# A mixture of experts on one core: the first quarter of the next slot's weights is split in two pieces between the copies of h

## The reference

```python
# x: 2304 x 512, w1: 8 x 512 x 1024, w2: 8 x 1024 x 512
logits = x @ w_gate
e_idx = np.argmax(logits, axis=1)          # one expert for each token
gate_w, eom = ...                          # a factor for each token
for e in range(8):
    mask = e_idx == e
    h = np.maximum(x[mask] @ w1[e], 0.0)
    out[mask] = gate_w[mask, None] * eom[mask, e, None] * (h @ w2[e])
```

## Time and profile before

| | |
|---|---|
| median of 3 runs | 1075.23 us (1075.14 to 1076.69) |
| the profiled execution | 1075.23 us, its span 1073.4 us |
| TensorE's mean granted clock in it | 0.982 of full speed |
| busy: PE, DVE, ACT, POOL | 95%, 57%, 56%, 43% of the span |
| third stage: slot 0 starts, slot 1 starts, last slot starts | 780.87, 796.05, 1052.14 us |

### The profile page before, as it was taken

The page is one execution under the profiler, slowest core; times in us unless marked ns, Lnnn a source line. Parts: engine busy times, 40 slices in busy tenths (PEclk is TensorE's granted clock), DMA queues, the critical chain, the costliest instruction groups (busy, mean ns, idle before and its releaser), DMA issues. The chain is left out here.

```text
span 1073.4 us, 19432 instructions
## 1 busy us (share of the span) xinstructions
PE 1017.6 (95%) x6901; PEld 840.3 (78%) x6901; DVE 612.5 (57%) x1137; ACT 596.3 (56%) x902; POOL 461.1 (43%) x725
## 2 busy tenths in 40 slices
PE   7999999999998999999999999999299999999996
PEld 5778778778776888888888888899177777777774
DVE  5788788888784334222422422332757777777773
ACT  4777787777774334222322322233168888877773
POOL 4777777777772000000000000000347777777773
PEclk9999999999999999999999999999589999999999
DMA  4322322323112110000000000010981554510110
GB/s 111 83 51 69 82 51 77 74 63 77 39 28 71 49 40 1 20 20 1 10 20 10 0 20 20 1 31 11 349 326 39 198 209 172 193 39 32 40 39 33
DMA packets 78891, 75.16 MB, mean 70 GB/s; under 512 B 49103, under 2 KB 59855, under 8 KB 78802
## 3 DMA queue, kind: packets, MB, share of 16 engines
q1 hardware_dynamic: 75282, 63.49, 19.7%
q0 software_dynamic: 3520, 10.49, 3.0%
HBM read 64.52 MB, written 10.49 MB: 70 GB/s over the span
## 5 line engine op out<-in xcount | busy, mean ns | idle before, releaser
L915 DVE TENSOR_TENSOR g_buf<-r_buf 128x512 f32<-128x512 f32 (+1 forms) x80 | 51.1, 639 | 236.1 <-ACT r_buf L853 236.1
L1165 POOL MEMSET ones<- 128x128 bf16 x1 | 0.2, 210 | 416.0 <-POOLq L652 416.0
L853 ACT ACTIVATE r_buf<-h_ps 128x512 f32<-128x512 f32 (+1 forms) x80 | 44.4, 556 | 240.0 <-PE h_ps L799 240.0
L1328 ACT ACTIVATE w_hi<-w_experts 128x2048 fp32r x88 | 161.1, 1906 | 13.2 <-issue 13.2
L1102 POOL TENSOR_TENSOR w_lo<-w_experts,w_hi 128x2048 fp32r<-128x2048 f32 x22 | 138.8, 6307 | 64.5 <-ACT w_hi L1328 64.5
L1102 DVE TENSOR_TENSOR w_lo<-w_experts,w_hi 128x2048 fp32r<-128x2048 f32 x66 | 149.1, 2286 | 28.0 <-ACT w_hi L1328 28.0
L478 ACT ACTIVATE e_sb<-s_sb,stats,live 128x576 f32<-128x576 f32 x144 | 124.5, 865 | 22.4 <-POOL stats L264 21.0
L799 PE MATMUL h_ps<-x_hi,w_in_hi 128*128 128x512 f32 (+1 forms) x320 | 120.2, 376 | 2.3 <-DVE x_lo L901 2.3
L799 PE MATMUL h_ps<-x_hi,w_in_lo 128*128 128x512 f32 (+1 forms) x320 | 118.6, 371 | 0.0
L799 PE MATMUL h_ps<-x_lo,w_in_hi 128*128 128x512 f32 (+1 forms) x320 | 118.5, 370 | 0.0
L816 PE MATMUL y_ps<-g_hi,w_out_hi 128*128 128x512 f32 (+1 forms) x320 | 117.9, 368 | 0.0
(11 more groups left out here) (190 smaller groups left out, 2228.3 us busy)
## 6 DMA issues: line engine op xcount, KB each, us to landing
w_experts<-in_moe_w_dram SPq DMA_DIRECT2D x16, 2048.0 KB, 9.6
y_rows<-y_row SPq DMA_DIRECT2D x36, 128.0 KB, 2.4
k_raw<-in_k_dram SPq DMA_DIRECT2D x32, 128.0 KB, 3.1
q_raw<-in_q_dram SPq DMA_DIRECT2D x32, 128.0 KB, 2.9
w_raw<-in_moe_w_in_dram SPq DMA_DIRECT2D x16, 256.0 KB, 3.1
v_nat<-in_v_dram SPq DMA_DIRECT2D x16, 256.0 KB, 2.6
y_T<-in_moe_w_out_dram SPq DMA_DIRECT2D x16, 256.0 KB, 2.6
v_odd<-in_v_dram SPq DMA_DIRECT2D x16, 64.0 KB, 2.3
```

What stands on the lines that cost most here:

```text
L915: V.tensor_tensor(g_buf[:, 0:cols], r_buf[:, 0:cols], r_buf[:, 0:cols], ALU.mult).then_inc(sq_done, 1)
L1328: nc.scalar.activation(group_of(w_hi, g), raw_group(buf, g), ACT.Copy).then_inc(hi_done, 1)
```

## The change

Group 0 is cut into two pieces of 128 x 1024 (blocks 0 and 1, blocks 2 and 3), so a slot's weights have five parts instead of four. On ScalarE the high part of piece 0 is made between the first relu and the copy of the first half of h, that of piece 1 between this copy and the second relu; groups 1 and 2 stay behind the copies, group 3 in front of the next slot's relu. On VectorE the low part of piece 0 is made right behind the low part of the first half of h, that of piece 1 where group 0 was. The waits count parts; TensorE's first products wait for both pieces. Its transposes of the second half of h go in front of the 5th product of group 2 instead of the 4th; those of the first half keep their place.

```diff
+PARTS = ((0, 0, 2), (0, 2, 4), (1, 0, 4), (2, 0, 4), (3, 0, 4))
+NPARTS = len(PARTS)
...
-        def split_lo(eng, alu, t, g, buf, done):
-            eng.wait_ge(hi_done, 4 * t + g + 1)
-            alu.tensor_tensor(group_of(w_lo, g), raw_group(buf, g), group_of(w_hi, g).bitcast(F32),
-                              ALU.subtract).then_inc(done, 1)
+        def split_lo(eng, alu, t, part, buf, done):
+            g, c0, c1 = PARTS[part]
+            eng.wait_ge(hi_done, NPARTS * t + part + 1)
+            alu.tensor_tensor(group_of(w_lo, g)[:, c0:c1], raw_group(buf, g)[:, c0:c1],
+                              group_of(w_hi, g)[:, c0:c1].bitcast(F32), ALU.subtract).then_inc(done, 1)
...
                 for g in range(2):
-                    pe.wait_ge(lo_dve, 3 * t + g + 2)
+                    pe.wait_ge(lo_dve, (NPARTS - 1) * t + g + 3)
-                    products(h_ps[g][:], x_hi, x_lo, 0, g, ahead_of=2 if g else None,
+                    products(h_ps[g][:], x_hi, x_lo, 0, g, ahead_of=6 if g else None,
                              between=lambda: h_transposed(t, 0)).then_inc(he_done, 1)
...
-                    products(oe_ps[p][:], h_hi, h_lo, 4 * g, 2 + g, ahead_of=None if g else 1,
+                    products(oe_ps[p][:], h_hi, h_lo, 4 * g, 2 + g, ahead_of=None if g else 4,
                              between=lambda: h_transposed(t, 1)).then_inc(y_done, 1)
...
-            def split_w(t, g, weights):
+            def split_w(t, part, weights):
                 buf, need = weights
-                if g % 2 == 0:
+                g, c0, c1 = PARTS[part]
+                if c0 == 0 and g % 2 == 0:
                     wait_first(act, w1_ready if g == 0 else w2_ready, need, act_on)
                 if not static(t) or t >= 1:
                     act.wait_ge(he_done if g < 2 else y_done, 2 * t - 1 + g % 2)
-                nc.scalar.activation(group_of(w_hi, g), raw_group(buf, g), ACT.Copy).then_inc(hi_done, 1)
+                nc.scalar.activation(group_of(w_hi, g)[:, c0:c1], raw_group(buf, g)[:, c0:c1], ACT.Copy).then_inc(hi_done, 1)
...
                 relu(t, 0)
+                if more:
+                    split_w(t + 1, 0, following)
                 split_h(t, 0)
+                if more:
+                    split_w(t + 1, 1, following)
                 relu(t, 1)
                 if more:
                     split_x(t + 1)
                 split_h(t, 1)
                 if more:
-                    split_w(t + 1, 0, following)
-                    split_w(t + 1, 1, following)
                     split_w(t + 1, 2, following)
+                    split_w(t + 1, 3, following)
...
                 split_h(t, 0)
                 if more:
+                    buf = weight_buffer(dve, t + 1)
+                    split_lo(dve, nc.vector, t + 1, 0, buf, lo_dve)
                     split_x(t + 1)
                 split_h(t, 1)
                 if more:
-                    buf = weight_buffer(dve, t + 1)
-                    split_lo(dve, nc.vector, t + 1, 0, buf, lo_dve)
                     split_lo(dve, nc.vector, t + 1, 1, buf, lo_dve)
+                    split_lo(dve, nc.vector, t + 1, 2, buf, lo_dve)
                 scale(t, p)
                 if more:
-                    split_lo(dve, nc.vector, t + 1, 2, buf, lo_dve)
+                    split_lo(dve, nc.vector, t + 1, 3, buf, lo_dve)
```

More of the change, by code:

```diff
@@ L1115, in load @@
                     end = sp.value_load(control[0:1, ENDS + e - BUFS:ENDS + e - BUFS + 1], min_val=0, max_val=SLOTS)
-                    wait_first(sp, lo_dve, 3 * end + 1, sp_on)
+                    wait_first(sp, lo_dve, (NPARTS - 1) * end + 1, sp_on)
                     wait_first(sp, lo_pool, end + 1, sp_on)
@@ L1162, in split @@
                 buf = weight_buffer(pool, t)
-                split_lo(pool, nc.gpsimd, t, 3, buf, lo_pool)
+                split_lo(pool, nc.gpsimd, t, NPARTS - 1, buf, lo_pool)
             nc.gpsimd.memset(ones[:], 1.0).then_inc(pool_set, 1)
@@ L1236, in products @@
                 for c in range(4):
-                    if c == ahead_of:
-                        between()
                     w = [x[:, g, c * 512:(c + 1) * 512] for x in (w_hi, w_lo)]
                     for n, (lhs, rhs) in enumerate(((lhs_hi, w[0]), (lhs_hi, w[1]), (lhs_lo, w[0]))):
+                        if 3 * c + n == ahead_of:
+                            between()
                         last = pe.matmul(out, lhs[:, c0 + c, :], rhs, start=(g != 3 and c == 0 and n == 0),
@@ L1268, in output @@
                     if g == 0:
-                        pe.wait_ge(lo_dve, 3 * t + 4)
+                        pe.wait_ge(lo_dve, (NPARTS - 1) * (t + 1) + 1)
                     else:
                         pe.wait_ge(lo_pool, t + 2)
-                    products(oe_ps[p][:], h_hi, h_lo, 4 * g, 2 + g, ahead_of=None if g else 1,
+                    products(oe_ps[p][:], h_hi, h_lo, 4 * g, 2 + g, ahead_of=None if g else 4,
                              between=lambda: h_transposed(t, 1)).then_inc(y_done, 1)
@@ L1327, in split_w @@
                     act.wait_ge(he_done if g < 2 else y_done, 2 * t - 1 + g % 2)
-                nc.scalar.activation(group_of(w_hi, g), raw_group(buf, g), ACT.Copy).then_inc(hi_done, 1)
+                nc.scalar.activation(group_of(w_hi, g)[:, c0:c1], raw_group(buf, g)[:, c0:c1], ACT.Copy).then_inc(hi_done, 1)
             def slot(t, first, more):
                 if not first:
-                    split_w(t, 3, (weight_buffer(act, t), None))
+                    split_w(t, 4, (weight_buffer(act, t), None))
                 if more:
@@ L1341, in slot @@
                 if more:
-                    split_w(t + 1, 0, following)
-                    split_w(t + 1, 1, following)
                     split_w(t + 1, 2, following)
+                    split_w(t + 1, 3, following)
             act.wait_ge(control_done, 1)
             weights = weights_of(0)
-            split_w(0, 0, weights)
-            split_w(0, 1, weights)
+            for part in range(3):
+                split_w(0, part, weights)
             split_x(0)
-            split_w(0, 2, weights)
-            split_w(0, 3, weights)
+            for part in range(3, NPARTS):
+                split_w(0, part, weights)
             slot(0, True, True)
@@ L1466, in slot @@
                 if more:
-                    buf = weight_buffer(dve, t + 1)
-                    split_lo(dve, nc.vector, t + 1, 0, buf, lo_dve)
                     split_lo(dve, nc.vector, t + 1, 1, buf, lo_dve)
+                    split_lo(dve, nc.vector, t + 1, 2, buf, lo_dve)
                 scale(t, p)
                 if more:
-                    split_lo(dve, nc.vector, t + 1, 2, buf, lo_dve)
+                    split_lo(dve, nc.vector, t + 1, 3, buf, lo_dve)
             buf = weight_buffer(dve, 0)
-            split_lo(dve, nc.vector, 0, 0, buf, lo_dve)
-            split_lo(dve, nc.vector, 0, 1, buf, lo_dve)
+            for part in range(3):
+                split_lo(dve, nc.vector, 0, part, buf, lo_dve)
             split_x(0)
-            split_lo(dve, nc.vector, 0, 2, buf, lo_dve)
+            split_lo(dve, nc.vector, 0, 3, buf, lo_dve)
             for t in range(RING):
```

## The result

The changed kernel takes 1079.90 us (median of 6 runs, 1078.69 to 1080.64) against 1075.18 us of the kernel before (6 runs): ratio 1.0042, 95% interval 1.0029 to 1.0055. It is **slower by 4.7 us**, where I had forecast 7.7 us less. The profiled execution took 1080.64 us, its span 1078.9. The loss lies in the third stage: slot 0 starts at 780.72 (780.87 before), the last slot at 1057.10 (1052.14). From slot 1 to slot 20 the period, from one slot's first product to the next one's, is 13.02 us in the mean, against 12.76.

What follows compares the result with a forecast made beforehand. TensorE was held at each slot's first product by VectorE's low parts of the weights. Removing the stall, -7.9 us, plus 0.2 at the last boundary gave -7.7: 1067.5 us, range 1065.6 to 1070.4.

Steps and rivals of the forecast that it cites:

- The old bound: Slot loop: transposes of h's second half, its ScalarE copy, `w_hi` group 0 (1.92 us), `w_lo` group 0 (2.30), next start.
- The price of the stall: TensorE's late starts between slots: 7.9 us lost over 20 boundaries, all of it to be recovered.
- The piece on ScalarE: High part of 1024 columns: 1.04 us, letting the copy of h in 0.3 us before it is wanted.
- the closest margin: Low part of h's second half, ready at 9.39, wanted at 9.54; 2 us in all kept for the upper end.
- (C): Rival: new code lengths turn loop back branches on TensorE's queue into fetches, losing 6 of 7.9 us: 1073.8 us, chance 0.05.
- (D): Rival: something the profile doesn't name holds TensorE's start, so early weights move nothing: 1075 us, chance 0.03.
- (B): Rival: ScalarE's pieces cost nearly as much as a whole group, delaying the second relu: 1090 us, slower, chance 0.05.
- one term: Piece 0's low part on VectorE: 1.22 us, from about 6.1 to 7.4 after the slot's start.
- the stretch of GpSimd: GpSimd's group 3 low part: bare 4.43 us, plus 1.0 per microsecond of VectorE's two-input weight work, 6.8 after the change.
- The consequence that I had excluded: VectorE's hole before the low part of x was taken as free, since nobody wants x before the next slot.
- Rival (A): GpSimd's loop over group 3 becomes the bound: 12.0 us, or 12.8 with a 7.6 piece, 1075 to 1077 us; chance 0.08.
- if TensorE waits for the low part of h at its third or fourth quarter: A listed sign of being wrong, beside GpSimd's piece over 7.1 us or a period over 12.5.

Runs made afterwards that it cites:

- the transposes alone: Kernel before, with only TensorE's transposes of the second half of h moved in front of the 5th product of group 2 instead of the 4th: 1079.53 us, ratio 1.0045.
- the order turned round: Changed kernel with piece 0's low part right before piece 1's, output scaled in four instructions before group 2's low part: 1133.15 us, ratio 1.0541.
- the low part late: Changed kernel, but VectorE makes piece 0's low part right in front of piece 1's, behind the second half of h's low part: 1066.10 us, ratio 0.9913.

## Why the prediction was wrong

**Right.** The old bound: the loop over transposes, ScalarE, VectorE and the next start, shown by the transposes alone (+4.7 for +0.23 us a slot). The price of the stall: I summed 7.9 us; the kernels with ScalarE's pieces that leave nothing out and that don't put piece 0's low part behind a whole subtraction of GpSimd's gain 7.7 to 10.1, the one with the order turned round apart. Of the 8.8 us between the spans of before and of the low part late, 8.2 are 19 slots of 12.33 instead of 12.76. The piece on ScalarE: 1.05 us, between relu and copy, the copy 0.17 us after the piece's end. `w_hi` group 3 and GpSimd's start: 0.31 and 2.43 after the slot's first product at 873.51, where I had 0.27 and 2.4. Even the closest margin, 0.15 us for the low part of the second half of h, is 0.13 in the kernel with the low part of piece 0 late (ready at 878.89, loaded for at 879.02). TensorE starts its 20 slots without a gap, so rivals (C) and (D) fell; the piece's 1.05 us speaks against (B). The stall of the earlier trace rows did go in the changed kernel, too: at 20 starts, TensorE's stream keeps its own pace to 0.01 us.

**Wrong: one term.** "The low part of piece 0 runs on VectorE from about 6.1 to 7.4." It runs from 6.30 to 8.98 in slot 7. I priced it by its columns (1.22 us), from rows in which nothing ran beside VectorE that had started earlier: in the old kernel VectorE's group 2 starts at 875.23, GpSimd at 875.62, and groups 0 and 1 run while GpSimd has no subtraction. From the same rows I took the stretch of GpSimd, 1.0 us for each microsecond of VectorE's, and did not ask what that slope says the other way round. A slope of 1.0, with VectorE at its usual 2.28, means that GpSimd stands still meanwhile; the trace of before only showed the order in which it is GpSimd that waits. The change was the first to start VectorE's subtraction in the middle of GpSimd's. The Trainium skill has this (SBUF — State Buffer, Who interferes with whom): in its words for the two-port modes, whoever issues first gets the shared pair, and the other fully blocks; issue order decides. The trace agrees for subtractions with two inputs, by the 2.68 us here and the 6.48 us of the order turned round. I had quoted that section for GpSimd alone.

**The consequence that I had excluded.** I said that nobody wants the low part of x before the next slot, so the hole in front of it is free. But VectorE works in order, and the low part of the second half of h stands behind it. I named its margin as the closest one and gave it 0.1 us a slot at the upper end. Piece 0 is 1.46 us longer than priced and leaves it ready at 883.68. TensorE's load before it went at 882.65, so it was wanted at 882.88 and went at 883.81, 0.93 later:

```profile
882.65 0.19 PEld L1245 LDWEIGHTS oe_ps<-w_hi,h_T_lo 128*128 128x128 f32 x1
883.81 0.19 PEld L1245 LDWEIGHTS oe_ps<-w_hi,h_T_hi 128*128 128x128 f32 x1 [0.97 <-issue]
```

The matmul starts lose 0.81 us by it (882.87 to 884.14, less two steps of 0.229). In each of 19 slots the changed kernel needs 0.69 us more in the mean than the 12.33 of TensorE's own work, where the kernel before needed 0.43. The new wait is larger than the one that it replaced, and the difference, 0.26 a slot or 4.9 us in all, is the loss. What should have stood in the sum is this margin against the longest form of the piece, held until GpSimd ends.

**Rival (A)** had the right loop in part and the wrong member. GpSimd's piece did not grow to 7.6; it shrank to 5.3 to 5.5, since group 2's low part lies beside it for only 1.0 us in slot 7, and piece 0, which starts behind it, doesn't stretch it. The loop closes over VectorE and its queue: 13.17 us instead of my 12.0.

I had listed "if TensorE waits for the low part of h at its third or fourth quarter" among the signs of being wrong. That is what the trace showed.

## What to carry to other kernels

When work is moved into a hole of an engine, look at what the other engines run during that hole and in which order the two will start, not only at how long the hole is. Where a trace shows one engine stretched by another at a slope of 1, price the turned order as well: in these kernels the later one waited for the whole rest of the earlier instruction, and all that was queued behind it waited too. If the two must overlap, start the engine that others wait for first, or cut the other's instruction, since the hold ended with it here; and do only the half of a split that the critical path needs, here ScalarE's.

## What the runs showed of the hardware that I had not expected

- Two subtractions with both inputs in SBUF, one on VectorE and one on GpSimd, do not share: the one that starts later does almost nothing until the other ends. GpSimd first by 0.27 us: 4.59 and 6.48 us. VectorE first by 1.09 us: 2.28 and 5.67. A lead of 0.13 us is enough, and in slot 4 of the kernel with the low part of piece 0 late 0.05 is.
- A copy on VectorE from SBUF to SBUF is held as well (2.15 us, of which 0.56 after GpSimd's end, against 0.69 to 0.70 where GpSimd runs no subtraction). A subtraction with one input in PSUM is not: 0.69 us beside GpSimd's and alone.
- The hold is for one instruction: with GpSimd's work in quarters the wait fell from 1.6 us to 0.65, and the quarter that came next was held in turn (2.28 us for a bare 1.1).
